# Second mixing of a token mixer: the up operand's load behind the last tokens, its split a batch later, three engines' loops written out, one seed of the down product sooner

## What is computed

```python
kv = einsum('bhsd,bhse->bhde', k, v)                 # attention without softmax
x  = rms_norm(einsum('bhsd,bhde->bhse', q, kv)) * g_norm
theta = x @ w_theta                                  # first mixing
y  = w_tok_r @ (x*cos(theta)) + w_tok_i @ (x*sin(theta))
u  = x + y;  x2 = u + relu(u @ w_ch)
h  = relu(x2.T @ w_tok1) @ w_tok2                    # second mixing: 576 -> 256 -> 576 tokens
u2 = x2 + h.T
out = u2 + relu(u2 @ w_ch1) @ w_ch2                  # up (512 -> 1536) and down product
```

## Time and profile before

| | us |
|---|---|
| median of 3 runs (1184.59 to 1185.31) | 1185.12 |
| the profiled execution, its own time | 1189.02 |
| its span, first to last instruction | 1187.2 |

### The profile page before, as it was taken

The page is one execution under the profiler, slowest core; times in us unless marked ns, Lnnn a source line. Parts: engine busy times, 40 slices in busy tenths (PEclk is TensorE's granted clock), DMA queues, the critical chain, the costliest instruction groups (busy, mean ns, idle before and its releaser), DMA issues.

```text
span 1187.2 us, 20987 instructions
## 1 busy us (share of the span) xinstructions
PE 1160.4 (98%) x7790; PEld 1120.1 (94%) x7790; DVE 850.6 (72%) x1243; ACT 480.4 (40%) x758; POOL 330.0 (28%) x210
## 2 busy tenths in 40 slices
PE   6999999999999999999998999999999999999998
PEld 5899999999899999899997999999999999999998
DVE  3977879797978878677564676666666786666664
ACT  3623324151424233234442455555556543333331
POOL 4462525444452524231551222223200000000000
PEclk9999999999999999999999999999999999999999
DMA  9614525151625230319996787766858999999983
GB/s 287 189 26 102 120 72 127 48 130 21 159 40 155 44 80 0 83 41 310 355 314 210 242 308 277 268 231 252 292 227 313 389 312 299 251 256 311 291 201 54
DMA packets 327245, 228.14 MB, mean 192 GB/s; under 512 B 231312, under 2 KB 295184, under 8 KB 326160
## 3 DMA queue, kind: packets, MB, share of 16 engines
q1 hardware_dynamic: 324784, 227.03, 62.6%
q10 hardware_dynamic: 2400, 0.30, 0.2%
HBM read 136.84 MB, written 92.80 MB: 193 GB/s over the span
## 4 chain that ended last, share of the span: by engine, by line
PE 65%; issue 15%; POOL 9%; DVE 6%; DMA 3%; ACT 2%; SPq 0%; POOLq 0%; DVEq 0%; ACTq 0%
PE bank L1368 9%; PE bank L1370 9%; PE bank L1369 9%; PE bank L43 7%; PE bank L45 7%; PE bank L44 7%; PE bank L371 4%; PE bank L365 4%; PE bank L366 4%; POOL z_z L956 3%; PE bank L310 2%; POOL z_z L958 2%; DMA z_g<-g_scratch 1%; POOL tokens_x_token_major L949 1%; POOL weights_rms_inverse L941 1%
## 5 line engine op out<-in xcount | busy, mean ns | idle before, releaser
L365 PE MATMUL bank<-weights_tok,z_z 128*128 128x288 f32 x576 | 165.0, 301 | 1.0 <-ACT z_z L591 1.0
L366 PE MATMUL bank<-weights_tok,z_z 128*128 128x288 f32 x576 | 161.3, 294 | 0.0
L371 PE MATMUL bank<-weights_tok,z_z 128*128 128x288 f32 x576 | 125.7, 296 | 1.1 <-POOL z_z L958 0.6
L365 PEld LDWEIGHTS bank<-weights_tok,z_z 128*128 128x128 f32 x576 | 108.1, 188 | 3.2 <-ACT z_z L591 2.4
L366 PEld LDWEIGHTS bank<-weights_tok,z_z 128*128 128x128 f32 x576 | 108.2, 188 | 0.0
L371 PEld LDWEIGHTS bank<-weights_tok,z_z 128*128 128x128 f32 x576 | 92.5, 187 | 3.0 <-POOL z_z L961 2.1
L941 POOL TENSOR_TENSOR weights_rms_inverse<-weights_mean_squares,weights_minus_half 128x8 f32<-128x8 f32 x40 | 65.5, 1639 | 95.2 <-DVE weights_mean_squares L724 95.1
L956 POOL TENSOR_TENSOR z_z<-tokens_cos,z_z 128x512 fp32r<-128x512 f32 x24 | 32.0, 1331 | 184.2 <-ACT z_z L589 184.2
L596 ACT ACTIVATE weights_x_channel_major<-attention_u 128x288 fp32r<-128x288 f32 x64 | 28.5, 445 | 126.0 <-DVE attention_u L791 126.0
L43 PE MATMUL bank<-weights_x_channel_major,weights_ch 128*128 128x288 f32 x256 | 77.3, 302 | 0.0
L45 PE MATMUL bank<-weights_x_channel_major,weights_ch 128*128 128x288 f32 x256 | 75.4, 294 | 0.0
(11 more groups left out here) (297 smaller groups left out, 3639.2 us busy)
## 6 DMA issues: line engine op xcount, KB each, us to landing
g_scratch<-attention_staged SPq DMA_DIRECT2D x36, 960.0 KB, 4.3
weights_g<-g_scratch SPq DMA_DIRECT2D x24, 1152.0 KB, 10.3
g_scratch<-attention_staged SPq DMA_DIRECT2D x36, 384.0 KB, 4.8
x_scratch<-attention_u SPq DMA_DIRECT2D x8, 1152.0 KB, 4.5
u_scratch<-attention_u SPq DMA_DIRECT2D x8, 1152.0 KB, 7.5
weights_raw_u<-u_scratch SPq DMA_DIRECT2D x6, 1536.0 KB, 7.6
qkv_u_left<-u_scratch SPq DMA_DIRECT2D x12, 768.0 KB, 9.5
x_tokens_scratch<-z_x_turned SPq DMA_DIRECT2D x112, 72.0 KB, 2.0
```

The source lines that it names most:

```text
L365: pe.matmul(out, x, wtok[0][:, zt, hs], start=(i == 0), stop=False)
L366: pe.matmul(out, x, wtok[1][:, zt, hs], start=False, stop=False)
L371: mm = pe.matmul(tok_bank(b, g)[:, 0:HALF], z[1][:, zt, c * P:(c + 1) * P], wtok[0][:, zt, half * HALF:(half + 1) * HALF], start=False, st ...
```

## The change

In four parts. ScalarE's and VectorE's loops of phase a, TensorE's and VectorE's of phase b are written out as straight code; the instructions in them stay. SP issues the up operand's load at n = 5 between the tokens and the store of u2, instead of at the end of n = 4. FIRST's split goes from batch 5 to batch 6 (VectorE: behind residual 5), SHARED's from batch 6 to batch 7 (VectorE: behind the hidden split, before the first residual); ScalarE's wait for `g_w` goes with it. In the down product's first group VectorE does `seed_e(0, 1)` before `c22(0, 0)` and the split behind it.

```diff
--- before.py
+++ after.py
@@ -691,7 +691,8 @@
                 for piece in range(3):
                     nxt["x_hi"](act, 0, piece)
         body(0, first=True)
-        loop(act, body, 1, B - 1)
+        for b in range(1, B - 1):
+            body(b)
         body(B - 1, more=False)
 
 
@@ -929,7 +930,8 @@
                 for c in range(1, NC):
                     turn_x2(b, c, turned_last)
         body(0, first=True)
-        loop(dve, body, 1, B - 1)
+        for b in range(1, B - 1):
+            body(b)
         body(B - 1, more=False)
 
 
@@ -1100,6 +1102,10 @@
                     sp.wait_ge(*prev["stored"])
                     sp.wait_ge(*prev["turned"])
                 load_tokens(sp, n + 2)
+            if n == B - 3:
+                sp.wait_ge(g_w, len(UP_ORDER))
+                sp.wait_ge(s_st, (B - 4) * DMA)
+                nxt["load"](sp, 0)
             sp.wait_ge(d_u, NG * (n + 1))
             sp.dma_start(u2_dram[:, :, n * S:(n + 1) * S], u2[:, :, :]).then_inc(s_st, DMA)
             if n == 0:
@@ -1110,10 +1116,6 @@
                 load(sp, n % 2, n + 2)
             if 1 <= n < NC:
                 store_last_turned(sp, n)
-            if n == B - 4:
-                sp.wait_ge(g_w, len(UP_ORDER))
-                sp.wait_ge(s_st, (B - 4) * DMA)
-                nxt["load"](sp, 0)
 
     def tensor(pe, nxt):
         def hidden(n):
@@ -1172,11 +1174,9 @@
         pe.wait_ge(d_tok, len(tok_weights))
         hidden(0)
 
-        def body(n):
+        for n in range(B - 1):
             mix(n)
             hidden(n + 1)
-        body(0)
-        loop(pe, body, 1, B - 1)
         mix(B - 1)
 
     def x_hi(act, n, piece):
@@ -1216,7 +1216,7 @@
             for step in range(len(UP_ORDER)):
                 if UP_BATCH[step] == n:
                     up_hi(step)
-            if n == B - 3:
+            if n == B - 2:
                 act.wait_ge(g_w, len(UP_ORDER))
             for k in PREP_HI.get(n, []):
                 nxt["prep_hi"](act, 0, k)
@@ -1264,6 +1264,8 @@
             hidden_lo(n, 1)
             if more:
                 x_lo(dve, n + 1, 0)
+            else:
+                nxt["prep_lo"](dve, 0, SHARED)
             for g in range(NG):
                 if more and g == 2:
                     x_lo(dve, n + 1, 1)
@@ -1275,16 +1277,15 @@
         def body(pair):
             batch(2 * pair, 0, pair)
             batch(2 * pair + 1, 1, pair)
-        body(0)
-        loop(dve, body, 1, PAIRS - 2)
-        body(PAIRS - 2)
+        for pair in range(PAIRS - 1):
+            body(pair)
         batch(B - 2, 0, PAIRS - 1)
         batch(B - 1, 1, PAIRS - 1, more=False)
 
     UP_ORDER = [FIRST, SECOND, LAST, LATE, SHARED, MIDDLE, THIRD]
     UP_BATCH = [0, 0, 1, 2, 3, 3, 4]
-    PREP_HI = {B - 3: [FIRST], B - 2: [SHARED], B - 1: [MIDDLE, SECOND]}
-    PREP_LO = {(B - 3, 4): FIRST, (B - 2, 4): SHARED, (B - 1, 2): MIDDLE, (B - 1, 4): SECOND}
+    PREP_HI = {B - 2: [FIRST], B - 1: [SHARED, MIDDLE, SECOND]}
+    PREP_LO = {(B - 2, 5): FIRST, (B - 1, 2): MIDDLE, (B - 1, 4): SECOND}
 
     def up_source(k):
 
@@ -2026,11 +2027,14 @@
                 out11(g, 1)
             out12(g, 0)
             out12(g, 1)
-            if g > 0:
+            if g == 0:
+                seed_e(g, 1)
+            else:
                 seed_e(g, 0)
             c22(g, 0)
             split(M + 7)
-            seed_e(g, 1)
+            if g > 0:
+                seed_e(g, 1)
             c22(g, 1)
             out22(g, 0)
             split(M + 8)
```

## The result

| | before | after |
|---|---|---|
| median of 20 runs on one chip, us | 1186.45 (1183.33 to 1188.98) | 1189.35 (1187.15 to 1191.95) |
| the profiled execution, its own time | 1189.02 | 1188.63 |
| its span | 1187.2 | 1186.8 |

The ratio is 1.0023, 95% interval 1.0015 to 1.0031: slower by 2.7 us, where 2.7 us faster was forecast. Measured again the ratio was 1.0011 (1.0001 to 1.0022). The two profiled executions don't show the loss: the one of after is 0.4 us shorter. So the traces tell where time went inside an execution, and the timed comparisons tell whether a version is faster.

A forecast was written before the change was run, and what follows sets the result against it. TensorE was taken as the bound, with little idle where edited. First stage 1.0, second mixing as a whole 0.4 and seed 1.3 sum to 2.7 us off 1185.12: 1182.4 us, range 1178.0 to 1185.6.

The forecast's parts named there:

- the steady iterations gain nothing: First stage, loops written out: no gain inside the steady batches, since TensorE is the bound there; 0 us.
- The exit itself: First stage, behind VectorE's loop: its 2.73 us "issue" stand goes and TensorE's wait for L762 with it; 1.0 us off.
- TensorE's exit: Last mixing of the second mixing stage: writing out the loop removes TensorE's "issue" stand; 1.6 us off, bounds 0 and 1.6.
- Rival 4: Both loop exits: their stands don't go or are met elsewhere, 2.6 us back, 1185.0 us; chance 0.07.
- The load and its splits: Second mixing: the 4.2 us stand before mixing 6 becomes 4.8 us inside it, waiting for the store of u2.
- the yardstick of batch 4: Second mixing: batch 4's store of u2 landed 10.4 us after its tokens went out, taken as base for batch 5.
- the price of 4.4 us: Second mixing: delay of batch 5's store of u2 by the operand's 1.57 MB ahead of it, from 4.1 to 5.5 us.
- The opening of the up product: Up product's start: the first MIDDLE matmul comes 9.75 us after the last mixing's start, held by splits and residuals.
- The 5.9 us of stand and clock: Second mixing before the change: 4.2 us lost by TensorE before mixing 6 and 1.7 us to the lower clock.
- The clock: Second mixing: the clock falls to 1.2 GHz behind the new stand as before; 1.7 us, bounds 0 and 1.7.
- The seed: Down product's first group: doing L1965 sooner removes TensorE's wait for it; 1.3 us off, bounds 1.1 and 1.3.

The follow-up runs named there:

- b_loops_only: Against before, only TensorE's and VectorE's loops of the second mixing written out: ratio 0.9994 (0.9984 to 1.0004).
- a_act_only: Against before, only ScalarE's loop of the first stage written out: ratio 0.9999 (0.9987 to 1.0012).
- load_last_seed: Against before, operand's load behind the store of u2 of batch 5, later splits, seed sooner, all loops kept: ratio 0.9968 (0.9956 to 0.9980).
- a_dve_only: Against before, only VectorE's loop of the first stage written out: ratio 0.9990 (0.9978 to 1.0002).
- a_dve_delay: VectorE's first-stage loop written out plus one copy of four numbers before L724 of each batch's second tile; against before, ratio 1.0013 (1.0003 to 1.0022).
- after_again: The changed kernel once more, no edit, timed against before: ratio 1.0011 (1.0001 to 1.0022).

## Why the prediction was wrong

- **The first stage, "the steady iterations gain nothing".** This is the step that failed. It put the term at nothing and never asked whether it could be a loss: the argument was that VectorE's instructions follow each other at the same distances in the unrolled batch. In fact they don't. Written out, VectorE starts again 0.18 us sooner behind its first wait for TensorE in the batch, GpSimd's gain comes 0.20 us sooner against TensorE, and that was enough to change which instruction meets it: the residual takes 1.59 us instead of 0.46. Cost: 0.39 us a batch, 2.3 us. The exit itself was right: forecast 1.0 us, in the trace 0.97, and VectorE's 2.73 us of "issue" is gone.
- **TensorE's exit, 1.6 us.** The stand went, as the profile should show. That it was the loop's price isn't borne out: it goes with any edit. And a gain from it isn't seen in the times: b_loops_only came out 0.7 us faster, a_act_only 0.1 us; their intervals reach to 1.9 and 1.5 us faster, so 1.6 us isn't quite ruled out. Rival 4, at 0.07, comes nearest to this.
- **The load and its splits.** Right in mechanism and in place: VectorE waits for the store of u2 (forecast 4 to 5 us, 4.77), a new wait for L1259, and the lower clock behind it. The store landed 639.9 - 626.2 = 13.7 us after its tokens were issued instead of 14.8, so the stand was 3.7 us instead of 4.8. Against batch 4 (10.4 us) the operand ahead of the store cost it 3.3 us instead of 4.4; against the same store in load_last_seed (9.8 us) it cost 4.0. The window at the stand shows 419 GB/s, at which 1.57 MB take 3.7 us. So the yardstick of batch 4 was 0.6 us too long, and the price of 4.4 us was 0.4 too high. The opening of the up product fitted: TensorE's first MIDDLE matmul came 9.82 us after the last mixing's start (649.83 to 659.65), forecast 9.75.
- **The size of what was given up.** The 5.9 us of stand and clock were those of one execution, the costliest of three. Set against the executions of unmoved loads without the exit's stand (a_dve_only, a_act_only, b_loops_only, a_dve_delay: mean 31.8 us), the four with the moved load have 33.1: the move costs 1.3 us. The forecast without its 1.6 us for the exit said 1.2. So this term was right, and its sign was hidden by counting the exit in it. (Set against before itself, whose three stretches hold the exit's stand, the moved load looks 0.8 us better in the traces.)
- **The clock.** It fell in all but two of the executions looked at. It didn't in load_last_seed, which has no stand, and not in a_act_only, where TensorE waited 3.2 us for L1246. So a stand of that length doesn't always bring it, and 1.7 us is the price of most executions, not of all. The mean granted clocks on record for the timed executions say how often. One fall of 3.4 us makes the mean 0.9986; 20 of 119 executions of before have 1.000, so no fall, and their medians lie 2 to 4 us below those of the rest; of the four kernels with the load ahead of the store 1 of 56 has. At 0.997 and less, so with about two falls, are 19 of 119 and 18 of 56. That is, as an estimate from these counts, 0.3 falls more in each execution, 0.5 us, which the sum below doesn't have.
- **The seed.** Forecast 1.3 us. From the first to the last of TensorE's 36 matmuls of that piece it took 7.46 to 7.52 us in the nine traces without the edit and 6.07 in the five with it: 1.4 us. Right. The three pieces ahead of it took 18.9 to 19.5 us without the edit and 19.0 to 19.6 with it (after has a wait of 0.3 us for L1961 there), so what is added there can't be put down to the seed.

Put together with what held: 2.3 - 1.0 for the first stage, 1.2 for the load, -1.3 for the seed, nothing for TensorE's exit: 1.2 us slower. The two comparisons gave 2.7 (1.8 to 3.7) and 1.3 (0.1 to 2.6). It agrees with the second and stays 0.6 us below the interval of the first; the estimate of 0.5 us for the more frequent falls of the clock would take up most of that.

**Open.** The traces of after are not longer than those of before (1186.8 and 1186.7 against 1187.2, 1187.2, 1186.3), although the timed runs are. All three traces of before have the exit's stand and one fall of the clock. Whether the stand is rarer in its other executions nothing here can show; that the fall is, the mean clocks above show. From the start of mixing 1 to group 6 of mixing 5 it took 57.8 us on average in the five executions with the second mixing's loops out, and 57.0 in the nine with them, but b_loops_only has 57.0 and its time isn't longer; the waits for the store of u2 in them vary from run to run. Eight of the eleven timed executions of b_loops_only have no fall of the clock, and their median, 1186.3 us, is 0.8 us above that of the seven such executions of before in the same comparison. Whether written-out code costs something there wasn't settled.

## What to carry to other kernels

Where an engine has slack, its instructions still have a phase against the others: before an edit makes it a little quicker, ask which instructions will move and which a wait holds in place, look for instructions that run two to three times longer than the same kind elsewhere (1.55 against 0.46 us), ask which one is next to be held up, and who waits for it. A large load goes into a queue behind everything that is needed sooner; ahead of the tokens it made tokens and store late, ahead of the store the store alone, and behind both it gained 5 us in its stretch. Price a stall on several executions of the same program before counting it as a gain, and don't put down to a loop a stand that the next edit anywhere might remove.

## What the runs showed of the hardware

- An instruction of VectorE with two SBUF inputs waits for the end of an instruction of GpSimd that started 0.00 to 0.01 us before it: 1.59 us instead of 0.46. Where VectorE started 0.19 us before (before, 143.43 and 143.62) it kept its 0.46 us, and GpSimd took 1.42 instead of 1.28 us.
- VectorE's first L789 of a batch, behind a wait for TensorE, came 1.98 to 1.99 us behind TensorE's L365 inside the loop and 1.80 to 1.81 us in straight code; from L724 to L732 VectorE took 0.17 to 0.18 us inside the loop and 0.11 in straight code; six times of six in each trace. Why the loop's instructions come later isn't shown.
- TensorE's stand of 1.3 to 2.1 us in the last mixing was in 3 of 3 executions of one program and in 0 of 6 executions of programs with the same TensorE loop but another edit.
- Straight code has small stands too: 0.3 us of "issue" once on VectorE in each of a_dve_only, a_dve_delay, after and after_again. The loop's exit has 2.6 to 3.1.
- A store of 1.18 MB took 7.5 us to land with only the tokens ahead of it, and 11.4 us with a load of 1.57 MB between.
